# Batch 0 of a gated linear attention: key scaling on GpSimd, a new order of loads, logarithms and copies

## The chip, the cores and the metric

The kernel runs on one core of one Trainium2 chip. The metric is the device time of one execution in microseconds. Before the change the median of 3 runs is 568.0 us (567.95 to 569.58).

## What is computed

Three stages follow one another on 4 batches of 768 tokens with 8 heads of 48 channels (384 channels in all). The reference, cut to what matters:

```python
# 1. gated linear attention, per batch and head
f = 1 / (1 + exp(-f_logit))
state = f[t] * state + outer(k[t], v[t])      # 48 x 48
y[t] = q[t] @ state
# 2. four experts of causal softmax attention, the best two of them weighted per token
logits = x @ w_gate; q, k, v = x @ wq[e], x @ wk[e], x @ wv[e]
out += w[e] * (softmax(causal(q @ k.T / 8)) @ v @ wo[e])
# 3. mixing
theta = x @ w_theta
u = x + w_tok_r @ (x * cos(theta)) + w_tok_i @ (x * sin(theta))
out = u + relu(u @ w_ch)
```

## The kernel before

**Layout.** Tokens are cut into 6 chunks of 128 (`NT`). In the recurrence channels lie on the partitions: two heads make a pair, in partitions 0 to 63 and 64 to 127, and there are 4 pairs. The gates f become a running sum of log(1 + exp(-f_logit)) over each chunk of 128 tokens; q is multiplied by exp(-sum), k by exp(+sum). Then each chunk needs scores k x q with a triangular mask (`keep`), outputs from the masked scores and V, outputs from the state and q, and an increment of the state. The state is carried by VectorE in two buffers.

**Batch 0 is loaded in three parts** of 256 tokens (`PARTS`, `part(n)`), two chunks each, for all pairs at once. SyncE's queue issues, in this order: gates of parts 0, 1, 2; q and k of part 0; woT and w_theta (0.96 MB); q and k of part 1; all of V; q and k of part 2; the weights of the expert layer (lines 378 to 405). The gates of batch 1 are issued once the keys of all parts are scaled (`k_scaled`, line 368 and after), q, k and V of batch 1 once the last outputs of batch 0 are done.

**ScalarE** (lines 637 to 663): three exponentials, three logarithms, then for part 0 and part 1 a copy of the sums, exp(-sum) (`shrink_first`, line 644) and exp(+sum) (`grow_first`, line 648). Exponential and logarithm need a table load between them. Then it copies the product wo x w_theta out of PSUM (line 661). In the chunk loop (`recurrence_copies`) it copies turned keys (line 673) and outputs (line 681) out of PSUM; part 2's exponentials stand in chunk 2, the splits of wq, wk, wv into a high part (`hi`, line 596) in chunk 3, the first gates of batch 1 (line 533) behind the last chunk.

**VectorE**: it clamps the gates (line 992), scans parts 0 and 1 (line 883), scales q and k of part 0 and q of part 1 (lines 890 and 896). Then come mask 0 (line 1007), k of part 1, and for each chunk c a mask of chunk c + 1, a sum (line 1024) and a scaling (line 1028) of the state; the scan of part 2 is in chunk 0, its q and k in chunk 1. In chunk 3 it waits for `worst_all`, forms the flag `steep` (line 1051: has any chunk decayed so far that a slow exact path is needed?) and reads it into a register, and masks the last chunk behind that. Four clamps of batch 1's gates (line 869) end the recurrence.

**GpSimd** builds constants, runs one partition_all_reduce on a constant (line 472), then the all-reduce of the largest decay (line 451, `worst_over_rows`), then the low parts of the split weights (`lo`, line 470): wv and the gate weights behind the last state (`s_ready`), wq and wk behind the clamps. In later batches it scales q and k (lines 464 and 467) ahead of that batch's all-reduce.

**TensorE**: twelve products wo x w_theta (line 1301), scores of chunks 0 and 1 (line 1271), then, once V is there, keys turned (line 1316), outputs (lines 1354 and 1358), increments (line 1339), chunk by chunk, the scores of a chunk one step ahead of the outputs of the chunk before. Then the outputs are transposed (line 1497), and the expert layer starts with products of three terms (lines 1253 to 1255): 6 tiles of wv and gate, which need `wvg_lo`, then 8 of wq and wk.

Engines are tied only by semaphores; each engine's own order is that of the program.

```python
            def worst_over_rows(b):
                pool.wait_ge(worst_here, upto(b, 1, 1))
                settle(pool, ticks)
                nc.gpsimd.partition_all_reduce(worst_of_all[:, :], worst[:, :], P,
                                               bass.bass_isa.ReduceOp.max).then_inc(worst_all, 1)
```

## Time and profile before

| | us |
|---|---|
| median of 3 runs | 568.0 |
| the profiled execution | 570.03 |
| its span, first to last instruction | 568.3 |
| TensorE busy | 538.7 (95%) |
| VectorE busy | 371.8 (65%) |
| ScalarE busy | 298.1 (52%) |
| GpSimd busy | 132.0 (23%) |

All times below count from the first instruction of the profiled execution. A busy time is a sum over the whole span; whether an engine is late at one place is seen only in its timeline there. PE is TensorE, PEld its weight loads, DVE VectorE, ACT ScalarE, POOL GpSimd, and POOLq GpSimd's sequencer. "[3.57 <-ACT ...]" behind a row is idle time ahead of it and what ended it; "issue" means that the profile shows nothing the engine waited for.

### The profile page before, as it was taken

The page shows a single profiled execution, that of the slowest core. Times are in us where ns is not written, and L with a number is a line of the kernel's source. Part 1 is how long each engine was busy: PE and PEld are TensorE (multiplying, and loading weights), DVE is VectorE, ACT ScalarE, POOL GpSimd, SP SyncE. Part 2 cuts the span into 40 slices and gives each one's busy share as a digit, 9 for nine tenths or more (in the row PEclk, how much of TensorE's full clock was granted, in tenths as well). Part 3 has the DMA queues.
Part 4 walks back from the last instruction along what each step waited for, and adds up shares of the span by engine and source line. Part 5 has one row for each costly group of instructions (what it writes and reads, how often), then busy time and mean ns, then how long its engine had stood idle before and what let it go on. Part 6 is the DMA issues. An engine that isn't in the chain of part 4 may idle for free.

```text
span 568.3 us, 14108 instructions
## 1 busy us (share of the span) xinstructions
PE 538.7 (95%) x5996; PEld 508.8 (90%) x5996; DVE 371.8 (65%) x672; ACT 298.1 (52%) x599; POOL 132.0 (23%) x88
## 2 busy tenths in 40 slices
PE   0989999999999999999999999999999999999997
PEld 0688878999789997899978899999999999999997
DVE  2988888878788787775768677555236544462434
ACT  5758687775877548733568664324222433133311
POOL 2003046035510025200022357112211212022200
PEclk9999999999999999999999999999999999999999
DMA  8948013052210430003600000010001100020002
GB/s 289 321 151 301 7 27 86 7 196 112 76 39 3 159 151 2 2 2 104 233 1 2 1 1 2 0 57 29 0 1 43 42 1 1 14 71 1 1 1 83
DMA packets 17969, 37.24 MB, mean 66 GB/s; under 512 B 2160, under 2 KB 10608, under 8 KB 17392
## 3 DMA queue, kind: packets, MB, share of 16 engines
q1 hardware_dynamic: 17904, 36.32, 18.5%
q8 instruction: 47, 0.77, 0.6%
q14 instruction: 18, 0.15, 0.1%
HBM read 31.46 MB, written 4.72 MB: 64 GB/s over the span
## 4 chain that ended last, share of the span: by engine, by line
PE 79%; DVE 8%; ACT 7%; issue 3%; DMA 2%; SPq 1%; DVEq 0%; ACTq 0%
PE bank L1253 18%; PE bank L1254 18%; PE bank L1255 17%; ACT prob L728 5%; PE bank L1462 4%; PE bank L1271 4%; PE bank L1399 4%; PE bank L1316 3%; PE bank L1358 3%; PE bank L1354 2%; DMA OT<-w_theta 2%; PE bank L1339 2%; PE bank L1562 1%; DVE gate L875 1%; DVE nmax L1121 1%
## 5 line engine op out<-in xcount | busy, mean ns | idle before, releaser
L1253 PE MATMUL bank<-z_h,wt_h 128*128 128x384 f32 x288 | 97.7, 339 | 0.0
L1254 PE MATMUL bank<-z_l,wt_h 128*128 128x384 f32 x288 | 97.4, 338 | 0.0
L1255 PE MATMUL bank<-z_h,wt_l 128*128 128x384 f32 x288 | 96.5, 335 | 0.0
L728 ACT ACTIVATE prob<-bank,nmax 128x384 f32<-128x384 f32 (+5 forms) x96 | 60.3, 638 | 20.7 <-DVE nmax L1121 20.7
L524 POOL TENSOR_TENSOR trig<-trig,x 128x768 f32<-128x768 f32 x18 | 33.6, 1865 | 149.6 <-ACT trig L634 92.6
L1121 DVE TENSOR_REDUCE nmax<-bank 128x1 f32<-128x384 f32 (+5 forms) x96 | 54.9, 616 | 10.0 <-PE bank L1405 5.3
L967 DVE TENSOR_SCALAR turns<-bank 128x384 int32<-128x384 f32 x22 | 12.2, 556 | 74.1 <-PE bank L1255 74.1
L1253 PEld LDWEIGHTS bank<-z_h,wt_h 128*128 128x128 f32 x288 | 54.0, 188 | 0.6 <-issue 0.3
L1254 PEld LDWEIGHTS bank<-z_l,wt_h 128*128 128x128 f32 x288 | 54.1, 188 | 0.0
L1255 PEld LDWEIGHTS bank<-z_h,wt_l 128*128 128x128 f32 x288 | 54.0, 188 | 0.0
L843 ACT CAST uT_h<-bank 128x384 fp32r<-128x384 f32 x24 | 11.5, 479 | 78.6 <-PE bank L1562 78.6
L1462 PE MATMUL bank<-probT,Vm 128*64 128x128 f32 x672 | 42.0, 276 | 0.7 <-DVE probT L1141 0.2
L1462 PEld LDWEIGHTS bank<-probT,Vm 128*64 128x64 f32 x672 | 36.2, 137 | 2.9 <-DVE probT L1141 1.4
L626 ACT COPY x<-bank 128x384 f32<-128x384 f32 x24 | 11.6, 481 | 49.8 <-PE bank L1255 44.5
L1007 DVE TENSOR_TENSOR probT<-bank,keep 128x1024 f32<-128x1024 f32 x24 | 29.3, 1221 | 12.0 <-PE bank L1271 11.9
L1358 PE MATMUL bank<-V,probT 128*64 128x48 f32 x768 | 36.1, 219 | 0.4 <-DVE probT L1007 0.3
L1399 PE MATMUL bank<-qk_h 64*128 64x512 f32 (+3 forms) x128 | 26.2, 406 | 7.1 <-ACT prob L728 5.4
L1358 PEld LDWEIGHTS bank<-V,probT 128*64 128x64 f32 x768 | 32.2, 137 | 0.8 <-issue 0.6
L1253 PE MATMUL bank<-xT_h,wqk_h 128*128 128x384 f32 x96 | 32.9, 343 | 0.0
L1254 PE MATMUL bank<-xT_l,wqk_h 128*128 128x384 f32 x96 | 32.4, 337 | 0.0
L1255 PE MATMUL bank<-xT_h,wqk_l 128*128 128x384 f32 x96 | 32.4, 337 | 0.0
L1354 PE MATMUL bank<-S,q 128*64 128x96 f32 x320 | 28.8, 255 | 2.6 <-DVE S L1028 1.9
(177 smaller groups left out, 1398.5 us busy)
## 6 DMA issues: line engine op xcount, KB each, us to landing
V<-v SPq DMA_DIRECT2D x4, 1152.0 KB, 11.1
gate<-fT SPq DMA_DIRECT2D x12, 384.0 KB, 3.2
q<-qT SPq DMA_DIRECT2D x12, 384.0 KB, 6.2
k<-kT SPq DMA_DIRECT2D x12, 384.0 KB, 6.5
wt_raw<-w_tok SPq DMA_DIRECT2D x6, 768.0 KB, 8.5
out<-x SPq DMA_DIRECT2D x24, 192.0 KB, 1.9
gate<-fT SPq DMA_DIRECT2D x3, 512.0 KB, 5.1
q<-qT SPq DMA_DIRECT2D x3, 512.0 KB, 9.5
```

The source lines that it names most:

```text
L524: nc.gpsimd.tensor_tensor(trig[:, s % 2, :, :], trig[:, s % 2, :, :], x2[:, s:s + 1, :].broadcast_to([P, 2, D]), ALU.mult).then_inc(z_made, 1)
L728: nc.scalar.activation(prob[:, m % 2, r, at], bank[r][:, at], ACT.Exp, bias=nmax[:, m, k:k + 1], accum_out=den[:, m // 2, which, e:e + 1]) ...
L1007: nc.vector.tensor_tensor(Am[:, c % 2, :, :], bank[c % 2][:, :].rearrange("p (h t) -> p h t", h=H), keep[:, None, :].broadcast_to([P, H, P ...
L1121: nc.vector.tensor_reduce(nmax[:, m, k:k + 1], bank[r][:, columns_of(m, which)], X, ALU.max, negate=True).then_inc(max_done, 1)
L1253: nc.tensor.matmul(o, a_h, b_h, start=start, stop=False)
L1254: nc.tensor.matmul(o, a_h, b_l, start=False, stop=False)
L1255: return nc.tensor.matmul(o, a_l, b_h, start=False, stop=stop)
L1271: mm = nc.tensor.matmul(bank[c % 2][:, slot(h):slot(h) + P], k[r:r + 64, h // 2, at], q[r:r + 64, h // 2, at], start=True, stop=True)
L1354: nc.tensor.matmul(ps(out_bank(c))[own, h * HD:(h + 2) * HD], q[:, h // 2, c * P + own.start:c * P + own.stop], S[:, c % 2, h // 2, :], st ...
L1358: mm = nc.tensor.matmul(ps(out_bank(c))[own, h * HD:(h + 1) * HD], Am[:, c % 2, slot(h) // P, own], V[:, c, h * HD:(h + 1) * HD], start=(c ...
L1399: mm = nc.tensor.matmul(bank[r][:, lo_:hi_], x[rows, a, queries], y[rows, 2 + a, keys], start=fresh_bank and n == 0, stop=False, skip_grou ...
L1462: mm = nc.tensor.matmul(ps(values_bank(m))[64 * r:64 * r + 64, at], Vm[:, s, e * ED:(e + 1) * ED], probT[:, m % 2, r, n * P:(n + 1) * P], ...
```

## The change

All of it is in batch 0.

- SyncE issues woT and w_theta ahead of q and k of part 0, and V in two transfers (chunks 0 and 1, then 2 to 5), each with its own semaphore; TensorE waits for the first ahead of outputs 0 and for the second ahead of chunk 2's work. The first turn of keys no longer waits for V.
- ScalarE: exponentials of parts 0 and 1, their logarithms, then part 2's exponential; part 2's logarithm is in the chunk loop behind the first copy of turned keys; a tiny exponential stands at the end of chunk 1; part 2's exp(+sum) goes behind the copy of outputs in chunk 2. The copy of wo x w_theta goes behind part 1's exp(+sum).
- The keys of part 1 (one instruction) and of part 2 (two, one for each chunk) are scaled by GpSimd, ahead of its all-reduce. TensorE waits for the two chunks of part 2 separately.
- GpSimd splits wv and the gate weights once `judged` is set instead of at the last state.
- VectorE reduces the largest sum ahead of scaling q of part 2.

```diff
@@ -276,6 +276,7 @@
         worst = s1("worst", [P, 1])
         worst_of_all = s1("worst_of_all", [P, 1])
         warm = s1("warm", [P, 1])
+        loaded = s1("loaded", [P, 1])
         steep = s1("steep", [P, 1], I32)
         slow_f, slow_k, slow_q, slow_s, slow_v, slow_y = (slow[:, n, :] for n in range(6))
 
@@ -325,7 +326,7 @@
         slow_floored = sem("slow_floored")
         slow_blank, slow_v_in, slow_in, slow_exp = sem("slow_blank"), sem("slow_v_in"), sem("slow_in"), sem("slow_exp")
         slow_step, slow_turn, slow_pair = sem("slow_step"), sem("slow_turn"), sem("slow_pair")
-        v_in = sem("v_in")
+        v_in, v_first, k_early = sem("v_in"), sem("v_first"), sem("k_early")
         f_in, q_in, k_in = ([sem(f"{n}{p}") for p in range(PAIRS)] for n in ("f_in", "q_in", "k_in"))
         w_in = [sem(f"w_in{i}") for i in range(7)]
         w_hi, wqk_lo, wvg_lo, late_lo = sem("w_hi"), sem("wqk_lo"), sem("wvg_lo"), sem("late_lo")
@@ -374,7 +375,11 @@
                     sp.dma_start(k[:, p, :], kT[b, :, p, :]).then_inc(k_in[p], 16)
 
             def load_v(b):
-                sp.dma_start(V[:, :, :], v[b]).then_inc(v_in, 16)
+                if b < 1:
+                    sp.dma_start(V[:, 0:2, :], v[b][:, 0:2, :]).then_inc(v_first, 16)
+                    sp.dma_start(V[:, 2:NT, :], v[b][:, 2:NT, :]).then_inc(v_in, 16)
+                else:
+                    sp.dma_start(V[:, :, :], v[b]).then_inc(v_in, 16)
 
             def load_first_gates(n):
                 sp.dma_start(gate[:, :, part(n)], fT[0, :, :, part(n)]).then_inc(f_in[n], 16)
@@ -385,9 +390,9 @@
 
             for n in range(PARTS):
                 load_first_gates(n)
-            load_first_qk(0)
             sp.dma_start(staged(W_OT, 768), woT).then_inc(w_in[3], 16)
             sp.dma_start(staged(W_TH, 1152), w_theta).then_inc(w_in[3], 16)
+            load_first_qk(0)
             load_first_qk(1)
             load_v(0)
             load_first_qk(2)
@@ -470,9 +475,19 @@
                 nc.gpsimd.tensor_tensor(dst, src, dst_hi.bitcast(F32), ALU.subtract).then_inc(s, 1)
 
             nc.gpsimd.partition_all_reduce(warm[:, :], halfpi[:, :], P, bass.bass_isa.ReduceOp.max).then_inc(consts, 1)
+            pool.wait_ge(q_scaled, 2)
+            pool.wait_ge(grown, 2)
+            pool.wait_ge(k_in[1], 16)
+            nc.gpsimd.tensor_tensor(k[:, :, part(1)], k[:, :, part(1)], gate[:, :, part(1)], ALU.mult).then_inc(k_scaled, 1)
+            pool.wait_ge(q_scaled, 3)
+            pool.wait_ge(grown, 3)
+            pool.wait_ge(k_in[2], 16)
+            for c, done in ((NT - 2, k_early), (NT - 1, k_scaled)):
+                at = slice(c * P, (c + 1) * P)
+                nc.gpsimd.tensor_tensor(k[:, :, at], k[:, :, at], gate[:, :, at], ALU.mult).then_inc(done, 1)
             worst_over_rows(0)
             pool.wait_ge(w_hi, 3)
-            pool.wait_ge(s_ready, NT - 1)
+            pool.wait_ge(judged, 1)
             lo(wvg_l[:, :, 0:256], wv_raw, wvg_h[:, :, 0:256], wvg_lo)
             lo(wvg_l[:, :, 256:260], graw[:, :, :], wvg_h[:, :, 256:260], wvg_lo)
             pool.wait_ge(clamped, gates(1, PAIRS))
@@ -648,19 +663,26 @@
                 nc.scalar.activation(gate[:, :, part(n)], gate[:, :, part(n)], ACT.Exp).then_inc(grown, 1)
                 decay_chunks(chunks_of(n))
 
-            for n in range(PARTS):
+            def exp_first(n):
                 act.wait_ge(clamped, n + 1)
                 nc.scalar.activation(gate[:, :, part(n)], gate[:, :, part(n)], ACT.Exp, scale=-1.0).then_inc(expf, 1)
-            for n in range(PARTS):
+
+            def log_first(n):
                 act.wait_ge(expf, n + 1)
                 nc.scalar.activation(gate[:, :, part(n)], gate[:, :, part(n)], ACT.Ln, bias=1.0).then_inc(logf, 1)
+
+            exp_first(0)
+            exp_first(1)
+            log_first(0)
+            log_first(1)
+            exp_first(2)
             shrink_first(0)
             grow_first(0)
             shrink_first(1)
+            grow_first(1)
             act.wait_ge(wth_mm, 1)
             nc.scalar.copy(staged(W_OTH, 768, 2), bank[2][:, :].rearrange("p (a n) -> p a n", a=2)[:, :, 0:D]
                            ).then_inc(wth_copied, 1)
-            grow_first(1)
 
             for it in range(B):
 
@@ -673,14 +695,20 @@
                             nc.scalar.copy(kTs[:, c % 2, :].rearrange("p (a h n) -> p h a n", h=2, n=64),
                                            bank[3][:, :].rearrange("p (h a n) -> p h a n", h=2, n=64)[:, :, 0:PAIRS, :]
                                            ).then_inc(kt_copied, 1)
+                        if it < 1 and c == 0:
+                            log_first(2)
                         if it < 1 and c == 2:
                             shrink_first(2)
-                            grow_first(2)
                         if c >= 1:
                             act.wait_ge(y_done, upto(it, NT, c))
                             nc.scalar.copy(xn[:, c - 1, :], ps(out_bank(c - 1))[:, 0:D]).then_inc(x_copied, 1)
                         if it < 1:
-                            if c == 3:
+                            if c == 2:
+                                grow_first(2)
+                            elif c == 1:
+                                act.wait_ge(consts, 13)
+                                nc.scalar.activation(loaded[:, :], halfpi[:, :], ACT.Exp)
+                            elif c == 3:
                                 act.wait_ge(w_in[0], 32)
                                 hi(wqk_h[:, :, :], staged(W_QK, 1536), w_hi)
                                 act.wait_ge(w_in[1], 32)
@@ -1009,8 +1037,6 @@
 
                 if it < 1:
                     mask(it, 0)
-                if it < 1:
-                    scale_first_k(1)
                 for c in range(NT - 1):
                     mask(it, c + 1)
                     if it < 1 and c % 2 == 0:
@@ -1033,9 +1059,8 @@
                         if c == 0:
                             scan_first(2)
                         elif c == 1:
+                            worst_sum(0)
                             scale_first_q(2)
-                            worst_sum(0)
-                            scale_first_k(2)
                         elif c == NT - 2:
                             for p in range(PAIRS):
                                 clamp_gates(1, p)
@@ -1265,7 +1290,12 @@
                         pe.wait_ge(k_scaled, gates(it, h // 2 + 1))
                     if it < 1 and c % 2 == 0 and h == 0:
                         pe.wait_ge(q_scaled, c // 2 + 1)
-                        pe.wait_ge(k_scaled, c // 2 + 1)
+                        if c < NT - 2:
+                            pe.wait_ge(k_scaled, c // 2 + 1)
+                        else:
+                            pe.wait_ge(k_early, 1)
+                    if it < 1 and c == NT - 1 and h == 0:
+                        pe.wait_ge(k_scaled, PARTS)
                     r = 64 * (h % 2)
                     at = slice(c * P, (c + 1) * P)
                     mm = nc.tensor.matmul(bank[c % 2][:, slot(h):slot(h) + P], k[r:r + 64, h // 2, at],
@@ -1360,17 +1390,21 @@
                                                   start=(c == 0), stop=(c == 0 or h % 2 == 1))
                     mm.then_inc(y_done, 1)
 
-                pe.wait_ge(v_in, upto(it, 16, 16))
                 if it >= 1:
                     pe.wait_ge(portion_copied, upto(it, len(TILES), 0))
                     pe.wait_ge(ot_done, upto(it, NT, NT - 2))
                 turn_k(0)
                 if it < 1:
                     pe.wait_ge(wth_copied, 1)
+                    pe.wait_ge(v_first, 16)
+                else:
+                    pe.wait_ge(v_in, upto(it, 16, 16))
                 outputs(0)
                 increments(0)
                 turn_k(1)
                 for c in range(1, NT):
+                    if it < 1 and c == 2:
+                        pe.wait_ge(v_in, 16)
                     if c + 1 < NT:
                         scores(it, c + 1)
                         if c + 2 < NT:
```

## Rows read from the trace of the kernel before

**Rows 1.** Windows of the whole run; columns: stretch, length, busy time (instructions), clock, DMA, GB/s

```profile
0.00:47.27 47.27, 29.64 (x519) 24.77 (x519) 33.12 (x49) 28.73 (x45) 8.37 (x22) 1.00 0.74 243
47.27:568.30 521.03, 509.11 (x5478) 484.06 (x5478) 338.73 (x624) 269.39 (x556) 123.63 (x67) 1.00 0.14 49
```

**Rows 2.** Timeline of TensorE, 14 to 48 us; columns: start, length, what, idle before

```profile
14.63 6.98 PE L1301 MATMUL bank<-OT 128*128 128x384 f32 x12 [14.63 <-DMA OT<-w_theta]
21.55 2.06 PE L1271 MATMUL bank<-q,k 64*128 64x128 f32 x32
...
25.96 1.11 PE L1271 MATMUL bank<-q,k 64*128 64x128 f32 x16
...
29.44 1.16 PE L1271 MATMUL bank<-q,k 64*128 64x128 f32 x16
...
42.00 0.39 PE L1354 MATMUL bank<-S,q 128*64 128x96 f32 x4 [1.04 <-DVE S L1028]
...
44.03 2.49 PE L1497 MATMUL bank<-ident,xn 128*128 128x128 f32 x18
47.27 0.39 PE L1253 MATMUL bank<-wvg_h,xT_h 128*128 128x260 f32 x1 [0.74 <-DVE xT_l L952]
```

**Rows 3.** Timeline of VectorE, 13 to 41 us

```profile
13.42 4.80 DVE L883 TENSOR_TENSOR_SCAN gate<-fresh,gate 128x256 f32<-128x256 f32 x8 [3.57 <-ACT gate L656]
...
23.90 1.22 DVE L896 TENSOR_TENSOR k<-k,gate 128x1024 f32<-128x1024 f32 x1
...
37.88 0.15 DVE L1051 TENSOR_SCALAR steep<-worst_of_all 128x1 int32<-128x1 f32 x1
39.57 1.22 DVE L1007 TENSOR_TENSOR probT<-bank,keep 128x1024 f32<-128x1024 f32 x1 [1.55 <-PE bank L1271]
```

**Rows 4.** Timeline of GpSimd, 15 to 45 us

```profile
15.17 0.38 POOL L472 PARTITION_ALL_REDUCE warm<-halfpi  x1 [11.00 <-issue]
32.66 1.13 POOL L451 PARTITION_ALL_REDUCE worst_of_all<-worst  x1 [17.11 <-DVE worst L901]
42.35 1.82 POOL L470 TENSOR_TENSOR wvg_l<-prob,wvg_h 128x768 fp32r<-128x768 f32 x1 [8.56 <-DVE S L1028]
44.14 0.52 POOL L470 TENSOR_TENSOR wvg_l<-graw,wvg_h 128x12 fp32r<-128x12 f32 x1
```

**Rows 5.** GpSimd's sequencer, one query by line each; columns: count, shortest/median/longest ns, first to last start

```profile
L472 POOLq MODIFY_POOL_CONFIG  x2: 13/13/13, 4.1 to 4.2; - x2
...
L451 POOLq MODIFY_POOL_CONFIG  x6: 3/11/11, 97.2 to 233.3; - x6
...
L470 POOLq MODIFY_POOL_CONFIG  x2: 83/83/83, 33.7 to 33.8; - x2
```

**Rows 6.** Timeline of GpSimd, 95 to 110 us

```profile
103.43 0.38 POOL L451 PARTITION_ALL_REDUCE worst_of_all<-worst  x1 [6.45 <-issue]
```

**Rows 7.** Windows of three stretches; the last two columns are DMA share and GB/s

```profile
5.00:15.00 10.00, 0.37 (x1) 0.40 (x2) 3.63 (x6) 7.20 (x7) 0.00 (x0) 1.00 1.04 356
15.00:24.00 9.00, 8.85 (x52) 5.34 (x51) 8.05 (x11) 7.33 (x14) 0.38 (x1) 1.00 1.07 374
...
97.00:103.40 6.40, 6.40 (x134) 6.00 (x133) 5.56 (x9) 4.75 (x8) 0.00 (x0) 1.00 0.25 68
```

**Rows 8.** Timeline of ScalarE, 10 to 28 us

```profile
10.95 1.28 ACT L656 ACT_TABLE_LOAD   x1
12.25 2.95 ACT L656 ACTIVATE gate<-gate 128x1024 f32<-128x1024 f32 x3
...
22.35 1.06 ACT L648 ACTIVATE gate<-gate 128x1024 f32<-128x1024 f32 x1
...
26.65 0.48 ACT L681 COPY xn<-bank 128x384 f32<-128x384 f32 x1
```

**Rows 9.** Line 869, 40 to 50 us; shortest/median/longest ns

```profile
L869 DVE TENSOR_SCALAR gate<-gate,floor x4: 606/611/2287, 41.8 to 45.0; 128x768 f32<-128x768 f32 x4
```

**Rows 10.** Line 1301, the products of w_theta; shortest/median/longest ns

```profile
L1301 PE MATMUL bank<-OT x12: 486/847/980, 14.6 to 21.1; 128*128 128x384 f32 x12
```

## Prediction, made before the changed kernel was run

> **What bounds the kernel now.** The whole-run view by windows comes first. TensorE works 509.1 of the 521.0 us after 47.27, but only 29.6 of the 47.3 before [rows 1]. The change touches the second stretch's first operand and everything ahead of it, so I ask one question: when does the long run of weight multiplications at line 1253 start? It is 47.27 now [rows 2]. From there TensorE is nearly always busy and nothing waits for a fixed time, so I carry every shift of that start to the end one for one.
>
> The TensorE timeline shows what leads there: the twelve products of w_theta from 14.63, waiting for a DMA; scores of chunks 0 and 1 at 21.55; scores of chunk 2 at 25.96 and of chunk 3 at 29.44; last outputs at 42.00; transposes at 44.03 [rows 2]. The VectorE timeline has scans from 13.42, the keys of part 1 at 23.90, the verdict "steep" at 37.88 and the last mask at 39.57 [rows 3]; four clamps of batch 1's gates follow, one of them of 2.29 us where the others take 0.61 [rows 9]. GpSimd looks empty: it reduces at 15.17 and 32.66 and splits weights at 42.35 [rows 4]. That emptiness is what the change wants to use, so its rows need a second look.
>
> **GpSimd isn't free.** The per-line view lists sequencer instructions too. A pair MODIFY_POOL_CONFIG stands ahead of the all-reduce of line 472 (at 4.1), ahead of the three later all-reduces of line 451 (97.2 to 233.3), and ahead of the first tensor_tensor behind an all-reduce (line 470, at 33.7) [rows 5]. The all-reduce at 32.66 has none: no other kind of work stands between it and line 472. So a pair comes where GpSimd changes between all-reduce and tensor_tensor. Its price in one direction shows: pair at 97.2, all-reduce at 103.43, 6.2 us, and GpSimd idle for 6.45 with "issue" as the reason [rows 5, 6]. At the start, with DMA share 1.04, pair at 4.1 and all-reduce at 15.17: 11.0 us; in the 6.2 us case the share was 0.25 [rows 4, 5, 7]. In the other direction the pair at 33.7 is hidden by a wait until 42.35, so that price lies between 0 and 8.6, or 11.0 under full DMA load. I take it as equal to the visible direction, the nearest row.
>
> The change puts three tensor_tensors between line 472 and the all-reduce of the batch. That makes one more change each way: a pair at 15.6 before the keys of part 1, and one between the last keys and the all-reduce, on whose result VectorE waits ("steep") before the last mask. The pair behind that all-reduce stays, but it now starts later, and its cover goes.
>
> **The change part by part.**
> - Weights ahead of q and k of part 0: 1.05 MB less before w_theta. At 356 GB/s [rows 7] that is 2.9 us, so TensorE starts at 11.7 instead of 14.63, and its 7.0 us [rows 2] end at 18.7. q and k of part 0 land by about 15, wanted at 15.9.
> - Part 2's exponential and logarithm later: the logarithms no longer wait for part 2's exponential, behind which the table load stood at 10.95 [rows 8]. ScalarE switches at 8.5, and the logarithms of 0.98 end at 10.8 and 11.8, so scans start at 10.9 instead of 13.42 and, at 2.4 a part [rows 3], end at 15.7. Two scalings of 1.2 [rows 3] give q and k of part 0 at 18.2: scores of chunks 0 and 1 at 18.7, 2.9 us earlier. Two more table loads of 1.28 [rows 8] lie where ScalarE waits, behind the first copy of turned keys (from about 21.6) and in chunk 1; cover: TensorE waits for keys of part 1 anyway. Without that cover, 0.5 us.
> - Keys of part 1 on GpSimd: 128x1024 at 1.82 us for 128x768 [rows 4] is 2.4. q of part 1 is scaled by 19.4, but the pair at 15.6 has to be over. Of its bounds 0 and 11.0 I take 10.2: DMA share is 1.07 to 24 [rows 7]; if 11.0 instead of 6.2 us is what such load does, 4.7 of the 6.2 are done by 24, and the rest takes about 1.8. So the keys run from 25.8 to 28.2. Scores of chunk 2 are at 28.2 against 25.96: 2.2 us late.
> - From there to the last keys: chunk 2's scores to chunk 3's are 3.5 us (25.96 to 29.44) [rows 2]; then copy 0.48 and part 2's growth 1.05 on ScalarE [rows 8], because the growth now stands behind the copy; then two key pieces of 128x512, 2.4 together; 0.3 of hand-overs. Last keys at 28.2 + 7.8 = 36.0.
> - All-reduce: pair at 36.1, 6.2 us, reduce 0.4: 42.7. The last mask was 1.7 us behind the start of "steep" [rows 3]: 44.5 against 39.57.
> - Last mask to the weight run. It was 7.7 us, 2.29 of them the slow clamp [rows 9], beside which GpSimd's split began at 42.35 [rows 4]. In the new order the split isn't there, but transposes then bound: 42.00 - 39.57 = 2.4, outputs 2.0, transposes 2.5, together 6.95: 51.4.
> - Weight split of line 470: behind the reduce, second pair 6.2, then 1.82 and 0.52 [rows 4]: 42.7 + 6.2 + 2.3 = 51.2. The weight run needs it, so both roads end at about 51.4, 4.1 us after 47.27. That the wait is now "judged" instead of the last state gains nothing.
> - TensorE's clock: granted is 1.00 throughout [rows 1], yet the twelve products have a median of 847 ns and a minimum of 486 [rows 10]: after idling to 14.63 it ran at the lower level (1.2 of 2.4 GHz) and rose near the end of the twelve. It would idle from 23.2 to 28.2. No row shows what a 5 us idle does to a busy engine, so bounds are 0 and ten products' worth of doubled time, 10 x 0.32 = 3.2. I take 0.8, since most of that stretch waits for ScalarE and VectorE.
> - V in two transfers: one more issue on SP of about 0.6; q and k of part 2 still land by 24 and are wanted at 30: nothing. Its first part lands at 18.5 and removes no wait that ends last. The copy of the product behind part 1's growth ends at 20.1, before mask 0 ends at 21: nothing. The tiny exponential: 0.2, hidden. Gates of batch 1 are issued behind the last keys at 36, land by 43, wanted at 46.9: hidden. VectorE loses two scalings of 1.21 us, worth nothing while it waits.
>
> Sum: 4.1 + 0.8 = 4.9 us. The profiled execution took 570.03 (span 568.3), 2.0 above the median of 568.0; it would become 574.9, and the median **572.9**.
>
> **Rivals.**
> - **A, loads not slowed by DMA.** Each config change costs 6.2 wherever it stands. Then keys of part 1 are there at 24.2, chunk 2's scores at 24.3, last keys at 33.0 (VectorE's chain then bounds), reduce over at 39.6, last mask at 41.3, weight run at 48.2: +1.0, 569.0. If only the visible direction costs, it is +0.5; if the change ahead of the reduce takes 8, between 6.2 and 11.0, beside the loads of batch 1's gates, it is +2.8. For it: the 11.0 may be a feature of the program's start. Against: full DMA load both times. The Trainium skill (GPSIMD Engine Reference, 2.1 Instruction dispatch) says that the first call to a freshly loaded kernel additionally pays about 6 us; the 6.2 agrees, the 11.0 doesn't, and by its figure alone the case is this one.
> - **B, faster: no config change on the path.** The place is the all-reduce: if GpSimd kept both kinds ready, the reduce would end at 33.5 and "steep" be decided by VectorE's chain. Then keys of part 1 end at 21.8, last mask at 36.7, weight run at 43.6: -3.6, 564.4. It decides as soon as all-reduce is over by 37.9, the old time of "steep". For: the emptiness of GpSimd. Against: three of three all-reduces behind tensor_tensors carry the pair [rows 5].
> - **C, slower still:** clock at the lower level through chunks 1 and 2 (the full 3.2) and config changes beside batch 1's gates at 8: +8, 576.
>
> **Chances.** Forecast's case (+2.8 to +6.5) 0.52; A 0.22; C 0.14; B 0.10; 0.02 elsewhere. About 0.3% (1.7 us) is what a measurement can tell from no change: A is mostly within it. Faster 0.10, same 0.14, slower 0.76. Range 568.2 to 576.2 holds A, the forecast's case and half of C.
>
> **What would show it.** Right: pairs of config on GpSimd near 15.6 and ahead of the reduce; keys of part 1 starting at 22 to 27 though q was scaled by 19.5; reduce some 6 us behind the last keys; "steep" past 41; weight run at 50 to 53. First scores at 18.7 tests the front. Wrong: keys of part 1 at 19.5, or reduce right behind the last keys; then the time falls below 566.

## The result: 1.5% slower, and where the profile after shows it

The changed kernel takes 576.81 us (median of 4 runs, 575.26 to 581.95); the kernel before took 568.17 in the runs beside it (4 runs, 567.95 to 569.58). The ratio is 1.0153, 95% interval 1.0127 to 1.0178. A later series of six runs gave 577.55 (575.2 to 581.1), ratio 1.015 (1.0123 to 1.0178). The forecast was 572.9 with a range up to 576.2: right in direction, too low by 3.9 us, and the result lies 0.6 us outside the range.

The profiled execution of the changed kernel took 575.26 us with a span of 573.5. First the page, to see where the difference lies: the engines, and two of the rows of 40 slices (PE is how busy TensorE is, PEclk the clock that it was granted, both in tenths).

```profile
span 573.5 us, 14122 instructions
PE 540.5 (94%) x5996; PEld 511.3 (89%) x5996; DVE 371.8 (65%) x670; ACT 300.8 (52%) x602; POOL 136.1 (24%) x91
PE   2786999999999999999999999999999999999997
PEclk9997999999999999999999999999999999999999
```

From the fifth slice on (57 us) TensorE is full and its clock is 9 everywhere. One slice of the clock is lower, the fourth, 43 to 57 us; before, the granted clock was 1.00 throughout [rows 1]. So everything that matters lies ahead of the long run of weight multiplications, called the weight run below. TensorE's timeline, with the same columns as [rows 2]:

```profile
11.43 6.60 PE L1331 MATMUL bank<-OT 128*128 128x384 f32 x12 [11.43 <-DMA OT<-w_theta]
17.96 2.06 PE L1301 MATMUL bank<-q,k 64*128 64x128 f32 x32
...
25.69 1.18 PE L1301 MATMUL bank<-q,k 64*128 64x128 f32 x16 [3.15 <-POOL k L481]
...
30.75 1.16 PE L1301 MATMUL bank<-q,k 64*128 64x128 f32 x16
...
47.34 0.59 PE L1384 MATMUL bank<-S,q 128*64 128x96 f32 x4 [6.18 <-DVE S L1054]
...
50.50 2.21 PE L1531 MATMUL bank<-ident,xn 128*128 128x128 f32 x18
52.58 0.36 PE L1278 MATMUL bank<-wvg_h,xT_h 128*128 128x260 f32 x1
```

The products of w_theta start 3.2 us earlier than before and so do, by 3.6 us, the scores of chunks 0 and 1. At chunk 2 (25.69) only 0.3 us of that is left, and TensorE has waited 3.15 us for the keys from GpSimd. Ahead of the last outputs it waits another 6.18 us, and the weight run starts at 52.58 instead of 47.27 [rows 2]: 5.3 us late. From its start to the end of the span it is 520.9 us, against 521.0 before. The shift was indeed carried one for one: span and profiled time are both 5.2 us longer.

GpSimd's timeline shows who holds the work back; "issue" in brackets means that the engine waited for nothing the profile shows:

```profile
15.05 0.57 POOL L477 PARTITION_ALL_REDUCE warm<-halfpi  x1 [10.88 <-issue]
23.21 2.33 POOL L481 TENSOR_TENSOR k<-k,gate 128x1024 f32<-128x1024 f32 x1 [7.59 <-issue]
32.43 2.52 POOL L487 TENSOR_TENSOR k<-k,gate 128x512 f32<-128x512 f32 x2 [6.89 <-ACT gate L663]
43.24 0.38 POOL L456 PARTITION_ALL_REDUCE worst_of_all<-worst  x1 [8.29 <-issue]
50.43 1.82 POOL L475 TENSOR_TENSOR wvg_l<-prob,wvg_h 128x768 fp32r<-128x768 f32 x1 [6.81 <-issue]
52.22 0.21 POOL L475 TENSOR_TENSOR wvg_l<-graw,wvg_h 128x12 fp32r<-128x12 f32 x1
```

Three gaps end in "issue": 7.59, 8.29 and 6.81 us. Before, the all-reduce at 32.66 started as soon as VectorE's sum was there, and the split at 42.35 waited for VectorE [rows 4]. The sequencer's rows of the same lines (count, shortest/median/longest ns, first to last start) put a pair of configuration changes at the head of each gap, answering to [rows 5]:

```profile
L481 POOLq MODIFY_POOL_CONFIG  x2: 83/83/83, 15.6 to 15.6; - x2
L456 POOLq MODIFY_POOL_CONFIG  x2: 20/20/20, 35.1 to 35.2; - x2
L475 POOLq MODIFY_POOL_CONFIG  x2: 83/83/83, 43.6 to 43.6; - x2
```

The instructions themselves take 83 or 20 ns; what they cost is the gap behind them. At the first of them nothing was missing: the keys of part 1 had landed at 17.3, their factors were ready at 18.4 and q was scaled at 18.8, 4.4 us before the keys. But not every pair has a gap behind it. One stands at the program's start, where GpSimd goes from memset to affine_select, and the next instruction starts at once:

```profile
L440 POOLq MODIFY_POOL_CONFIG  x2: 11/11/11, 2.4 to 2.5; - x2
...
2.53 0.29 POOL L440 TENSOR_SCALAR_AFFINE_SELECT ident<-ident 128x128 f32<-128x128 f32 x1 [0.49 <-POOL fresh L438]
```

So what costs time here is not the pair by itself but the change between tensor_tensor and all-reduce, called a switch below. VectorE's timeline, read against [rows 3], has the effect on the verdict "steep" and on the last mask, 44.92 instead of 39.57, and one thing more:

```profile
10.68 4.76 DVE L911 TENSOR_TENSOR_SCAN gate<-fresh,gate 128x256 f32<-128x256 f32 x8 [1.04 <-ACT gate L672]
...
23.29 4.55 DVE L911 TENSOR_TENSOR_SCAN gate<-fresh,gate 128x256 f32<-128x256 f32 x4 [0.48 <-ACT gate L672]
...
33.68 1.69 DVE L1054 TENSOR_TENSOR S<-Su,chunk_decay 128x384 f32<-128x384 f32 x1
...
37.21 0.56 DVE L1054 TENSOR_TENSOR S<-Su,chunk_decay 128x384 f32<-128x384 f32 x1
43.65 0.15 DVE L1076 TENSOR_SCALAR steep<-worst_of_all 128x1 int32<-128x1 f32 x1 [5.89 <-POOL worst_of_all L456]
44.92 1.22 DVE L1035 TENSOR_TENSOR probT<-bank,keep 128x1024 f32<-128x1024 f32 x1 [1.11 <-issue]
```

Eight scans took 4.76 us at the start; four took 4.55 beside the 2.33 us of keys on GpSimd. A scaling of the state that takes 0.56 took 1.69 beside the second keys.

The windows of six stretches give the granted clock, the first number after the five engines; the last two are DMA share and GB/s:

```profile
22.50:25.70 3.20, 0.06 (x4) 0.04 (x2) 2.72 (x2) 3.10 (x5) 2.33 (x1) 1.00 1.06 329
25.70:30.70 5.00, 5.00 (x88) 4.87 (x88) 4.97 (x9) 1.70 (x3) 0.00 (x0) 0.66 0.74 208
30.70:41.10 10.40, 10.40 (x260) 9.93 (x256) 6.15 (x7) 6.08 (x11) 2.52 (x2) 1.00 0.45 150
41.10:47.30 6.20, 0.06 (x3) 0.00 (x0) 2.50 (x5) 0.48 (x1) 0.38 (x1) 0.72 0.03 10
47.30:50.50 3.20, 3.16 (x48) 3.10 (x49) 2.02 (x4) 1.58 (x2) 0.07 (x1) 0.50 0.02 5
50.50:52.60 2.10, 2.10 (x21) 2.03 (x19) 0.80 (x2) 1.78 (x5) 2.10 (x3) 0.98 0.45 95
```

TensorE idles 3.2 us, then works a chunk at 0.66 of its clock; it idles 6.2 us, then works the last outputs at 0.50, the lower of its two levels, in 3.2 us instead of the 2.0 of before.

### The profile page after: what moved, and what is told of

It reads as the page before. It is cut to its first block, busy times and chain, and to the rows that moved or that the text cites. A ratio compares the mean times of both kernels' runs of the same rounds, so it can differ in the third digit from the quotient of the medians.

```text
span 573.5 us, 14122 instructions
## 1 busy us (share of the span) xinstructions
PE 540.5 (94%) x5996; PEld 511.3 (89%) x5996; DVE 371.8 (65%) x670; ACT 300.8 (52%) x602; POOL 136.1 (24%) x91
## 4 chain that ended last, share of the span: by engine, by line
PE 77%; DVE 8%; ACT 8%; issue 5%; DMA 1%; POOL 1%; DVEq 0%; SPq 0%; POOLq 0%
PE bank L1278 18%; PE bank L1279 17%; PE bank L1280 17%; ACT prob L756 5%; PE bank L1496 4%; PE bank L1433 4%; PE bank L1301 4%; PE bank L1346 3%; PE bank L1388 3%; PE bank L1384 2%; PE bank L1596 1%; PE bank L1369 1%; PE bank L1531 1%; DVE gate L903 1%; DVE nmax L1146 1%
## 5 line engine op out<-in xcount | busy, mean ns | idle before, releaser
L1388 PE MATMUL bank<-V,probT 128*64 128x48 f32 x768 | 37.3, 225 | 0.3 <-DVE probT L1035 0.3
L1384 PE MATMUL bank<-S,q 128*64 128x96 f32 x320 | 30.0, 265 | 7.0 <-DVE S L1054 7.0
L1388 PEld LDWEIGHTS bank<-V,probT 128*64 128x64 f32 x768 | 33.7, 144 | 0.6 <-issue 0.4
## 6 DMA issues: line engine op xcount, KB each, us to landing
V<-v SPq DMA_DIRECT2D x3, 1152.0 KB, 10.7
```

Source lines behind the costliest of these rows:

```text
L1384: nc.tensor.matmul(ps(out_bank(c))[own, h * HD:(h + 2) * HD], q[:, h // 2, c * P + own.start:c * P + own.stop], S[:, c % 2, h // 2, :], st ...
L1388: mm = nc.tensor.matmul(ps(out_bank(c))[own, h * HD:(h + 1) * HD], Am[:, c % 2, slot(h) // P, own], V[:, c, h * HD:(h + 1) * HD], start=(c ...
```

## Experiments

Each ratio is against the kernel before in the same series; its median there was 569.15, 569.03 and 568.64 in the three series (16, 11 and 11 runs). Diffs are against the changed kernel unless said otherwise. The first series holds the next four kernels.

**1. Keys back on VectorE, all the rest of the change kept.** The three products leave GpSimd's queue; VectorE scales the keys of part 1 behind the first mask and those of part 2 behind q of part 2, each as one operation.

```diff
-            pool.wait_ge(q_scaled, 2)
...
-            for c, done in ((NT - 2, k_early), (NT - 1, k_scaled)):
-                at = slice(c * P, (c + 1) * P)
-                nc.gpsimd.tensor_tensor(k[:, :, at], k[:, :, at], gate[:, :, at], ALU.mult).then_inc(done, 1)
...
+                if it < 1:
+                    scale_first_k(1)
...
+                            scale_first_k(2)
```

> The changed kernel with the keys of parts 1 and 2 scaled by VectorE again, everything else as changed. Theory S (the switches of GpSimd's configuration between all-reduce and tensor_tensor are the whole loss): no pair stands ahead of batch 0's all-reduce, first scores stay at 18.0, the last mask is near 37.5 and the weight run starts near 44.5, so 565.4 us, 2.8 below the kernel before. Rival T (the two more table loads of ScalarE and the new order of loads also cost): weight run not before 46.5, 567.5 us or more. Rival M (most of the loss has nothing to do with GpSimd): the time stays above 570.

Measured: 565.78 us (565.42 to 566.52), ratio 0.9939 (0.9917 to 0.9961). GpSimd's timeline of this kernel:

```profile
15.12 0.38 POOL L477 PARTITION_ALL_REDUCE warm<-halfpi  x1 [10.94 <-issue]
28.47 1.13 POOL L456 PARTITION_ALL_REDUCE worst_of_all<-worst  x1 [12.97 <-DVE worst L919]
36.94 1.82 POOL L475 TENSOR_TENSOR wvg_l<-prob,wvg_h 128x768 fp32r<-128x768 f32 x1 [7.33 <-issue]
```

The reduce follows its input at once; no pair stands ahead of it. Scores of chunk 2 start at 22.64, the last mask at 36.53, the weight run at 42.98. One edit turns 1.5% slower into 0.6% faster: the keys on GpSimd cost 577.55 - 565.78 = 11.8 us (medians of two series, whose kernel before differs by 0.1), and everything else in the change gains 3.4 (569.15 - 565.78; 3.0 in run 11).

**2. Kernel before, with the keys on GpSimd alone.** Against the kernel before: the three products and their waits added to GpSimd's queue, the two scalings taken from VectorE's, the scores' wait split as in the change; VectorE's sum `worst_sum(0)` stands ahead of q of part 2, also as in the change. Order of loads, logarithms, the two transfers of V and the wait ahead of the weights' split stay as before.

```diff
+            pool.wait_ge(q_scaled, 2)
...
+            nc.gpsimd.tensor_tensor(k[:, :, part(1)], k[:, :, part(1)], gate[:, :, part(1)], ALU.mult).then_inc(k_scaled, 1)
...
-                if it < 1:
-                    scale_first_k(1)
```

> The kernel before with this one part of the change: keys of parts 1 and 2 on GpSimd. Theory S: two more switches, near 15.6 and ahead of the all-reduce; the last mask waits for the all-reduce and is at 44 to 46, the weight run starts at 51.5 to 53.5, and the time is 573 to 577 us, that of the changed kernel, though the first scores are at 21.5: the gain of the other parts lies under the stall. Rival T: the time is nearer to the kernel before than to the changed one, under 571.

Measured: 574.85 us (574.56 to 576.08), ratio 1.0105 (1.0077 to 1.0133). All three gaps are there: pair at 15.28 and keys at 23.52, pair at 34.53 and reduce at 42.34, pair at 42.67 and split at 49.97. The first is free here, since without the earlier front the scores of chunk 2 start at 26.03, as before. So the keys on GpSimd alone make a loss of 5.7 us, and an early front only exposes the first gap too: the changed kernel, with its front 3 us earlier, is still 2.7 us slower than this one (577.55).

**3. The change without the first all-reduce**, whose result nobody uses.

```diff
-            nc.gpsimd.partition_all_reduce(warm[:, :], halfpi[:, :], P, bass.bass_isa.ReduceOp.max).then_inc(consts, 1)
```

> The changed kernel without the first all-reduce on a constant. Then GpSimd still holds what tensor_tensor needs when the keys of part 1 come, and only the switch ahead of batch 0's all-reduce is left. Theory S with each switch priced by where it stands: keys of part 1 at about 19, scores of chunk 2 at about 22.5, last keys at about 32, the all-reduce 8 us later at 40, last mask at 42, weight run at 49 to 50: 569.5 to 571.5 us. Were only the first switch to blame, it would be near 564.5; were only the second, at 575 as the changed kernel.

Measured: 571.96 us (571.31 to 576.39, ten of eleven within 573.7), ratio 1.0056 (1.0034 to 1.0079). Its GpSimd:

```profile
19.79 2.37 POOL L480 TENSOR_TENSOR k<-k,gate 128x1024 f32<-128x1024 f32 x1 [15.61 <-DVE q L917]
29.94 2.51 POOL L486 TENSOR_TENSOR k<-k,gate 128x512 f32<-128x512 f32 x2 [7.78 <-DVE q L917]
39.30 0.38 POOL L456 PARTITION_ALL_REDUCE worst_of_all<-worst  x1 [6.84 <-issue]
46.82 1.81 POOL L475 TENSOR_TENSOR wvg_l<-prob,wvg_h 128x768 fp32r<-128x768 f32 x1 [7.14 <-issue]
```

The keys of part 1 now start when q is scaled, 3.4 us earlier, and with no keys beside them the four scans take 2.44 us. So the gap ahead of the keys was a switch from the all-reduce, not a wait for data. Without it the median is 5.6 us lower, the profiled time 3.3 (575.20 of run 5 against 571.88). The median is 0.5 us above the range expected.

**4. Also no all-reduce in batch 0.** On top of 3, GpSimd copies each partition's own sum: the maximum over partitions is left out in batch 0.

```diff
+                if b < 1:
+                    nc.gpsimd.tensor_copy(worst_of_all[:, :], worst[:, :]).then_inc(worst_all, 1)
+                else:
+                    nc.gpsimd.partition_all_reduce(...)
```

> The changed kernel without the first all-reduce, and with batch 0's all-reduce replaced by a copy on GpSimd: this leaves out the maximum over the partitions in batch 0 (each row keeps its own). No switch is left in batch 0. Theory S: keys of part 1 end near 21.5, last mask at 36.7, weight run at 43.6, 564.4 us; what the change would bring if GpSimd needed no switch. Rival T: above 567 with no stall on GpSimd.

Measured: 565.96 us (564.43 to 566.89), ratio 0.9928 (0.99 to 0.9956). The last mask starts at 36.17 and the weight run at 42.27, 7.0 us earlier than in 3. Of this 2.0 us are lost again behind it (522.9 us from there to the end, against 521.0), most of it at the start of the next batch, where a clamp waited 2.43 us for the load of its gates and TensorE 1.59 us at 98.49; so the time is 1.6 above the 564.4 expected. The two later switches are worth 6.0 us of median, with that loss in it.

The second series asks what the rest of the excess is, starting with the changed kernel unchanged.

**5. The changed kernel again.**

> The changed kernel once more, unchanged, beside the others of this series. In its first profile three switches took 7.6, 8.1 and 6.8 us. If their length changes from run to run, the time scatters by about a microsecond and its median is between 575 and 577 us; the order of rows stays.

Measured: 577.55 us (575.2 to 581.1), 0.6 above the expected range, with a scatter of 6 us and not of 1. The profiled execution is again the shortest, 575.20. Two windows of it answer to the second and fifth of after:

```profile
25.85:29.40 3.55, 3.55 (x90) 3.43 (x90) 3.55 (x6) 2.11 (x5) 0.00 (x0) 1.00 0.80 230
...
46.30:49.40 3.10, 3.10 (x48) 3.02 (x48) 1.93 (x4) 1.58 (x2) 0.00 (x0) 0.50 0.02 5
```

After 2.7 us of idle, not 3.2, chunk 2 ran at full clock and took 3.5 us, not 5.1. Yet the last keys began only 0.95 us earlier than in the first profile: here the stretched scans set their time, since q of part 2 is scaled behind them. The last outputs are at 0.50 again, and this time the transposes are slow too (49.41 to 52.56, clock 0.60). The weights' split was done at 51.69, so here TensorE's own work alone set the start of the weight run, 52.56. Same program, two ways to the same 575.2.

**6. Sixteen extra products in the stall**, to keep TensorE busy; nobody reads them.

```diff
+                    if it < 1 and c == NT - 1:
+                        pe.wait_ge(kt_copied, NT - 1)
+                        pe.wait_ge(x_copied, 1)
+                        for n in range(16):
+                            nc.tensor.matmul(ps(7)[:, 0:D], ident[:, :], xn[:, 0, :], start=True, stop=True)
```

> The changed kernel with 16 more products of 128x384 on TensorE, into a free bank, in its stall ahead of the last outputs: their result isn't used. The first profile had the last outputs at the lower clock, 3.2 us instead of 2.0. Expected: they take 2.0 again. Theory S says that the end of the weight split on GpSimd (52.4) is the second of two roads to the weight run at 52.6, so that the time falls by 0.3 us at most. Rival K (the clock is what the forecast missed): it falls by 1.1 us or more.

Measured: 579.77 us (578.18 to 582.15), ratio 1.0185 (1.0159 to 1.0211). The products took 10.6 us and became the bound themselves, so the time, which was expected to fall and rose, says nothing of the clock's price. The outputs behind them took 1.7 us instead of 3.2, so the low clock was due to the idling.

**7. Loads of batch 1's gates behind the all-reduce.**

```diff
+                    if it < 1:
+                        sp.wait_ge(worst_all, 1)
```

> The changed kernel with the loads of batch 1's gates issued behind batch 0's all-reduce instead of behind the last keys. If those loads lengthen the switch, the pair at 35.2 is over after 6.2 to 6.9 us instead of 8.1 and the last mask comes 1.2 to 1.9 us earlier; the following switch then shares its time with the loads and grows by as much, so the weight run gains 0.5 us at most and may lose 1. Rival: a switch takes 8 whatever is loaded beside it.

Measured: 576.02 us (574.15 to 579.3), ratio 1.0115 (1.0084 to 1.0145). Windows of the two switches, ahead of the reduce and behind it, in this kernel:

```profile
35.40:41.10 5.70, 5.70 (x153) 5.46 (x152) 2.50 (x4) 3.06 (x5) 0.00 (x0) 1.00 0.02 3
...
41.40:49.90 8.50, 4.06 (x55) 3.90 (x53) 4.79 (x8) 2.65 (x4) 0.11 (x2) 0.68 0.60 196
```

and in the changed kernel:

```profile
35.10:43.30 8.20, 6.06 (x159) 5.69 (x156) 2.51 (x4) 3.55 (x6) 0.06 (x1) 1.00 0.58 194
...
43.50:50.40 6.90, 3.06 (x48) 3.09 (x48) 4.52 (x8) 1.58 (x2) 0.12 (x1) 0.52 0.01 4
```

The loads moved from one switch to the other, and the length moved with them: 8.1 to 5.7 us ahead of the reduce, 6.8 to 8.4 behind it. The last mask came 2.15 us earlier (42.77), but the weight run starts at 52.85. The longer third switch isn't why, as the split was done at 51.85. TensorE's clock was: after 3.74 us of idling it was at the lower level through outputs and transposes, and the transposes took 3.7 us instead of 2.1.

**8. The maximum over partitions by TensorE.** Both all-reduces of batch 0 go, and nothing is left out: TensorE turns the column of sums into a row of one partition, VectorE takes its maximum, and the verdict is read from that partition.

```diff
-            nc.gpsimd.partition_all_reduce(warm[:, :], halfpi[:, :], P, bass.bass_isa.ReduceOp.max).then_inc(consts, 1)
...
-            worst_over_rows(0)
...
+                            pe.wait_ge(worst_here, 1)
+                            pe.wait_ge(s_sum, c - 1)
+                            nc.tensor.transpose(ps(5)[0:1, D:D + P], worst[:, :], ident[:, :]).then_inc(worst_all, 1)
...
+                        nc.vector.tensor_reduce(worst_of_all[0:1, :], ps(5)[0:1, D:D + P], X, ALU.max).then_inc(worst_turned, 1)
```

> The whole change, but batch 0's maximum over the partitions is made by a transpose on TensorE into PSUM and a reduce of one row on VectorE; both all-reduces of batch 0 are gone, and nothing is left out. No switch stands in batch 0. Expected as in the run with the own row, plus 0.3 us for the reduce: last mask 36.5, weight run 42.6, 564.5 to 566 us, below the kernel before and level with or up to 1 us below the run with the keys on VectorE.

Measured: 564.78 us (564.53 to 566.85), ratio 0.9929 (0.9908 to 0.9949). The timeline of GpSimd, then that of VectorE:

```profile
19.13 2.38 POOL L480 TENSOR_TENSOR k<-k,gate 128x1024 f32<-128x1024 f32 x1 [14.94 <-DVE q L916]
29.29 2.52 POOL L486 TENSOR_TENSOR k<-k,gate 128x512 f32<-128x512 f32 x2 [7.78 <-DVE q L916]
34.81 1.84 POOL L475 TENSOR_TENSOR wvg_l<-prob,wvg_h 128x768 fp32r<-128x768 f32 x1 [2.99 <-DVE steep L1079]
```

```profile
33.29 0.27 DVE L1047 TENSOR_REDUCE worst_of_all<-bank 1x1 f32<-1x128 f32 x1
...
34.53 0.13 DVE L1079 TENSOR_SCALAR steep<-worst_of_all 1x1 int32<-1x1 f32 x1
35.77 1.22 DVE L1033 TENSOR_TENSOR probT<-bank,keep 128x1024 f32<-128x1024 f32 x1 [1.10 <-PE bank L1304]
```

Every gap of "issue" in batch 0 is gone; the maximum costs 0.27 us on each of two engines. The weight run starts at 41.86, 10.7 us earlier than in the changed kernel. With the switches gone, keys on GpSimd are no loss.

The third series mends the flawed experiment 6 and repeats the two best.

**9. Nine extra products instead of sixteen.**

```diff
-                        for n in range(16):
+                        for n in range(9):
```

> The changed kernel with 9 more products on TensorE in its stall ahead of the last outputs, result unused (the 16 of the run before were 10.6 us and became the bound). 9 x 0.66 is 5.9 us in a stall of 6.3. The last outputs then take 2.0 us instead of 3.2. Theory S+K (two roads end together; the clock is a price in those executions in which it stays low longer): profiled weight run no more than 0.3 us earlier, because the weight split ends at 52.4; median over the runs 1 to 2 us lower than the changed kernel's 577.5, and scatter smaller. Theory S alone: median unchanged within 0.5 us.

Measured: 577.69 us (575.98 to 582.05), ratio 1.0157 (1.0123 to 1.0192); the profiled execution took 579.16. Its GpSimd shows why that one was long:

```profile
15.71 3.63 POOL L477 PARTITION_ALL_REDUCE warm<-halfpi  x1 [11.52 <-issue]
26.89 2.33 POOL L481 TENSOR_TENSOR k<-k,gate 128x1024 f32<-128x1024 f32 x1 [7.55 <-issue]
```

The first reduce took 3.63 us instead of 0.38 to 0.83, and all behind it came later. The last outputs ran at full clock, in 1.7 us (51.3 to 53.0), and the transposes in 2.2 from 53.02, but the weight run began at 56.48, once the split ended at 56.34. Here the full clock bought nothing, since the third switch ends as late. The median is within 0.2 us of run 5's: of the two expectations, the one that gives the clock no price held.

**10. Nine products, and the split of the values' weights on VectorE**, in its own wait for the reduce.

```diff
-            lo(wvg_l[:, :, 0:256], wv_raw, wvg_h[:, :, 0:256], wvg_lo)
-            lo(wvg_l[:, :, 256:260], graw[:, :, :], wvg_h[:, :, 256:260], wvg_lo)
...
+                    if it < 1 and c == NT - 3:
+                        dve.wait_ge(w_hi, 3)
+                        lo(wvg_l[:, :, 0:256], wv_raw, wvg_h[:, :, 0:256], wvg_lo)
```

> As the run with 9 products, and the split of wv and of the gate weights is made by VectorE while it waits for the all-reduce. Now neither GpSimd's third switch nor the lower clock stands ahead of the weight run. Expected: weight run at 51.0 to 51.7 in the profile, 1 to 1.5 us earlier than with the 9 products alone, 573.5 to 575 us. If the third switch never was a second road, no difference from the 9 products alone.

Measured: 576.74 us (574.06 to 579.71), ratio 1.0142 (1.0106 to 1.0178). The split takes 0.95 us on VectorE. From last mask to weight run it is 6.30 us (47.51 to 53.81), against 7.66 in the changed kernel, 8.73 in run 5 and 7.89 in run 9. With both roads freed 1.4 us or more are won in that stretch; the split moved by itself was not run. The weight run was expected at 51.0 to 51.7 and the time at 573.5 to 575: what came before ate the gain, as first reduce (0.83), first switch (8.5) and second (8.3) were all long in the profiled execution.

**11 and 12. Experiments 1 and 8 again, side by side.**

> The changed kernel with the keys on VectorE once more, to compare it with the next on the same chip: 565.5 to 566.0 us.

> The whole change with the maximum made by TensorE and VectorE, once more: 564.5 to 565.5 us, 0.5 to 1.3 below the run with the keys on VectorE (its last mask was 0.8 and its weight run 1.1 us earlier in the profile).

Measured: 565.62 us (565.31 to 565.81), ratio 0.9938 (0.9918 to 0.9959), and 564.92 (564.47 to 565.14), ratio 0.9925 (0.9905 to 0.9945). The ranges of these six runs each don't overlap: the version without all-reduces in batch 0 is faster by 0.7 us and the best found.

## Why the prediction was right in direction and too low

**What bounds.** Right: the start of the weight run is the measure of everything (+5.3 there, +5.2 at the end).

**The front.** Right within 0.7 us: products at 11.43 (forecast 11.7), scans at 10.68 (10.9), first scores at 17.96 (18.7). Experiments 1 and 11 price it, with the other small parts: 3.0 to 3.4 us once the switches don't eat it.

**The first switch.** Pair at 15.6 as foreseen, keys at 23.21 instead of 25.8. The term of 10.2 us was mis-sized: 7.6, and 7.4 to 9.1 over the seven profiles with this switch. I had built it from the 11.0 us at the start, which was no guide to a switch in the middle of the same load; and by its own terms 1.5 of the 6.2 us were left at 24, not 1.8, which would make it 9.9. Chunk 2 was 2.5 us earlier than forecast.

**From chunk 2 to the last keys.** Forecast 7.8 us, measured 9.3 (25.69 to 34.95). Two costs the steps had at nothing: the clock in the first profile (chunk 2 took 5.1 us instead of 3.5), and the scans stretched beside the keys, which alone hold q of part 2 back in run 5. "VectorE loses two scalings, worth nothing" missed that GpSimd's products take time back from it.

**The second switch.** Forecast 6.2 us, taken from the one in [rows 6] where the DMA share was 0.25; it took 8.1 at a share of 0.58, 8.0 in run 5. Rival A named this case ("if it takes 8 beside the loads of batch 1's gates") and I priced it apart from the forecast instead of in it. Experiment 7 points to the load: without the gates' transfers beside it the same switch took 5.7. The errors nearly cancel: last mask at 44.92, forecast 44.5.

**Last mask to weight run.** Forecast 6.95 us, measured 7.66. No slow clamp and no split in between, as foreseen; but outputs at the lower level took 3.2 us instead of 2.0, and the transposes 2.1 instead of 2.5. The only stall I had given a clock cost was the one ahead of chunk 2; I had put TensorE to sleep for 6 us ahead of the last outputs myself, and priced the awakening at nothing. The split's road, forecast to end at 51.2, ended at 52.43, level with the other. So in this execution a faster clock alone would have won 0.15 us at most, and run 9 shows no gain from it; in run 5's, where the split was done at 51.69, it could have won 0.9.

**The sum** for the profiled execution was 574.9; it took 575.26 and, in the second profile, 575.20. That step held, though by terms that cancel: start of chunk 2 -2.5; from there to the last keys +1.5; from these to the end of the reduce 8.7 instead of 6.7, +2.0; to the last mask 1.3 instead of 1.8, -0.5; to the weight run +0.7; and -0.8 for the clock, which the measured pieces hold already. Together +0.4.

**The step that failed** is the last: "it would become 574.9, and the median **572.9**". I subtracted the 2.0 us by which the profiled execution of the kernel before lay above its median. Of the changed kernel the profiled execution lies 1.6 below its median (575.26 against 576.81), in the second series 2.3 below. That is 3.6 of the 3.9 us missed. An excess of one execution is not a constant of the measurement but that execution's own luck. What the change does to the luck: it puts the first reduce and the first switch on the path while the loads run. In the profiles that reduce took 0.38 to 3.63 us and the switch 7.4 to 9.1.

Three more profiles show this, since up to "steep" runs 6, 9 and 10 have the same work on this path as the changed kernel. "Steep" starts there at 45.61, 47.33 and 45.81, against 43.65 and 42.57 in the two profiles of the changed kernel: the middle one of the five lies 2.0 us behind the first profile, where the medians lie 1.6 and 2.3 above the profiled times. What came late were the first reduce (3.63 us in run 9), the first switch (9.1 in run 6, 8.5 in run 10) and, against run 5, chunk 2, which in all three took 5.1 to 5.6 us at a lowered clock, as in the first profile.

With the first reduce and the first switch out of the way (experiment 3) the median stands at the profiled time, 571.96 against 571.88; with all switches gone six runs lie within 0.7 us in experiment 12 and within 2.3 in experiment 8. Experiment 2, where chunk 2 hardly waits for the first switch, has 1.5 us of scatter and its median at the profiled time. How much each part adds to the longer runs stays open, since runs without a profile show no timeline: at the same mean clock of 0.991 the second series has both 575.2 and 577.6, so the clock alone isn't it.

**The rivals.** A (6.2 for every change) fell, though for the first switch it was nearer: keys of part 1 done at 25.5, where it said 24.2 and the forecast 28.2. B fell: each change between the two kinds of work carried its pair, in both directions. What it got right is the price: with the switches taken out the time is near its 564.4 (564.78 and 564.92 in runs 8 and 12). C was nearest, 576: its switch of 8 us beside the gates came true, and its low clock in part, 1.6 us in chunk 2 of the first profile and 1.2 in the last outputs, where it had 3.2 in chunks 1 and 2. Its terms add up to 9.1 us (4.1 + 3.2 + 1.8), so it should have said 577.

## What to carry to other kernels

An engine's empty row is not free time: look at its sequencer for what it must do between one kind of work and another, and count such a switch on both sides of an operation moved in between work of the other kind. A cross-partition maximum on the critical path was cheaper here as a transpose and a reduction (0.27 us each) than as an all-reduce that needs a switch. And don't carry the excess of one profiled execution over its median to another kernel: where a change puts something of varying length on the path, the median can move away from the profile.

## What the hardware showed that was not expected

**The switch costs in both directions, and more beside transfers.** From tensor_tensor to all-reduce it took 5.6 to 6.2 us at a DMA share of 0.02 or less (run 7, and the last batch of every kernel), 5.7 to 5.9 at 0.14 or 0.15 (the third batch), 6.0 to 6.7 at 0.22 to 0.27 (the second) and 6.9 to 8.3 at 0.57 to 0.68. Back to tensor_tensor it took 6.8 to 7.3 at 0.00 to 0.05, 8.4 at 0.60 (run 7) but 7.4 at 0.72 (run 1; 7.3 in run 11), and 7.4 to 9.1 at 0.99 to 1.07. So transfers beside it lengthen it as a rule, and the share alone doesn't give its length. The Trainium skill (GPSIMD Engine Reference, 2.1 Instruction dispatch) gives approximately 6 us for the first call to a freshly loaded kernel. The changes to an all-reduce beside few transfers agree with it; those beside more transfers and those back were longer, and these runs show a price at every change between the two kinds that the engine had no wait to hide. Between all-reduce and all-reduce there is none (run 1: 28.47).

**The first all-reduce** took 0.38 us in four profiles, 0.57 to 0.83 in five, and 3.63 in one. In the kernel before nobody waited for it.

**The clock.** In chunk 2 the granted clock was 1.00 after 2.7 us of idling in one execution (run 5) and 0.66 after 3.2 us in another; the chunk took 3.5 us there and 5.1 here, and 5.1 to 5.6 in runs 6, 7, 9 and 10, after 3.1 to 6.7 us. After 6.2 and 6.5 us of idling it was 0.50, the 1.2 GHz level, for the next 3.1 us in both profiles of the changed kernel; in run 5 it was 0.60 for 3.2 us more. The price here was 1.2 us of outputs, and in run 5 also 1.1 us of transposes.

**VectorE beside GpSimd.** Four scans took 4.55 and 4.11 us beside the keys and 2.44 apart from them; the scaling of the state 1.69 and 1.38 instead of 0.56. The Trainium skill (SBUF — State Buffer, Who interferes with whom) says that a VectorE instruction with two SBUF inputs contends with a GpSimd instruction that reads SBUF; scan and scaling have both inputs there, and the trace agrees. The masks, whose first input is a PSUM bank, kept their 1.2 us.
